# Attention and two mixtures of experts on one core: the second routing, its order on three engines, and the fourth sub-tiles' transfers

## The reference

```python
x = attention(q, k, v)                       # 1536 tokens x 512
# first mixture: top 2 of 8, D=512, F=1024
noisy = x @ w_gate + log1p(exp(x @ w_noise)) * noise
out[mask] += top2_w[mask, k, None] * (relu(x[mask] @ w1[e]) @ w2[e])
# second mixture: top 1 of 8
logits = x @ w_gate + modality_bias[modality_id]
e_idx = argmax(logits); gate_w = softmax(logits)[e_idx]
out[mask] = gate_w[mask, None] * (relu(x[mask] @ w1[e]) @ w2[e])
```

## Time and profile before

| what | us |
|---|---|
| median of 3 runs | 687.44 |
| lowest, highest | 685.09, 689.46 |
| the profiled execution | 682.12 |
| its span, first to last instruction | 680.2 |
| TensorE busy | 645.6 |
| VectorE, ScalarE, GpSimd busy | 322.6, 276.2, 185.5 |
| mean granted TensorE clock | 0.982 |

### The profile page before, as it was taken

One profiled execution on the slowest core, in us unless ns is written; L12 is line 12 of the kernel. 1 busy time (PEld: TensorE's weight loads), 2 busy tenths in 40 slices (PEclk: granted clock), 3 DMA queues, 4 the chain that ended last, 5 costly groups with the idle time before them and its releaser, 6 DMA issues.

```text
span 680.2 us, 11358 instructions
## 1 busy us (share of the span) xinstructions
PE 645.6 (95%) x3872; PEld 585.2 (86%) x3873; DVE 322.6 (47%) x651; ACT 276.2 (41%) x529; POOL 185.5 (27%) x194
## 2 busy tenths in 40 slices
PE   7989999899999999999999999999499999999993
PEld 6989999898999999999999998998278888788873
DVE  4466646587465527254452724353775422452211
ACT  5668866442444234253433523232245221441210
POOL 2500100117361633516153331101531212111101
PEclk9999999999999999999999999998599999999997
DMA  7877822255584545656364511510894510010100
GB/s 207 277 238 244 284 74 68 91 220 134 197 231 162 110 146 154 188 155 172 116 140 151 154 20 22 159 53 8 221 375 156 175 42 31 35 31 32 47 16 27
DMA packets 52096, 91.23 MB, mean 134 GB/s; under 512 B 8591, under 2 KB 14735, under 8 KB 52048
## 3 DMA queue, kind: packets, MB, share of 16 engines
q1 hardware_dynamic: 41872, 69.21, 30.1%
q0 software_dynamic: 10176, 21.38, 13.9%
HBM read 74.52 MB, written 18.40 MB: 137 GB/s over the span
## 4 chain that ended last, share of the span: by engine, by line
PE 83%; DVE 6%; DMA 3%; ACT 2%; issue 2%; SPq 1%; ACTq 0%; POOL 0%; DVEq 0%; POOLq 0%
PE banks L984 6%; PE banks L983 6%; PE banks L992 6%; PE banks L925 5%; PE banks L926 5%; PE banks L928 5%; PE banks L730 5%; PE banks L758 4%; PE banks L1234 4%; PE banks L1239 4%; PE banks L1235 4%; PE banks L1260 4%; PE banks L1261 4%; PE banks L1264 3%; PE banks L742 2%
## 5 line engine op out<-in xcount | busy, mean ns | idle before, releaser
L603 POOL DMA_INDIRECT x_moe<-rows,dst_idx x29 | 57.8, 1994 | 157.5 <-DVE rows L2067 111.2
L1679 DVE TENSOR_TENSOR split<-stage,split 128x2048 fp32r<-128x2048 f32 x32 | 73.3, 2290 | 42.4 <-ACT split L1326 42.3
L925 PE MATMUL banks<-xTs,split 128*128 128x416 f32 (+1 forms) x256 | 88.9, 352 | 2.0 <-issue 2.0
L926 PE MATMUL banks<-xTs,split 128*128 128x416 f32 (+1 forms) x256 | 86.4, 342 | 0.0
L983 PE MATMUL banks<-hTs,split 128*128 128x416 f32 x224 | 80.0, 357 | 0.0
L984 PE MATMUL banks<-hTs,split 128*128 128x416 f32 x224 | 78.6, 351 | 0.0
L1461 ACT ACTIVATE hTs<-banks 128x416 fp32r<-128x416 f32 x56 | 29.0, 518 | 85.0 <-PE banks L928 85.0
L1326 ACT ACTIVATE split<-stage 128x2048 fp32r<-128x2048 f32 x32 | 60.9, 1907 | 0.7 <-DMA stage<-w1a 0.7
L1581 ACT ACTIVATE hTs<-banks 128x512 fp32r<-128x512 f32 x28 | 16.6, 597 | 108.2 <-PE banks L1249 108.2
L928 PE MATMUL banks<-xTs,split 128*128 128x416 f32 (+1 forms) x256 | 56.3, 341 | 0.0
L730 PE MATMUL banks<-k_sb,q_sb 128*128 128x260 f32 (+2 forms) x192 | 50.0, 387 | 3.4 <-DMA k_sb<-k_w 2.0
(11 more groups left out here) (306 smaller groups left out, 1330.0 us busy)
## 6 DMA issues: line engine op xcount, KB each, us to landing
stage<-w1a SPq DMA_DIRECT2D x16, 1024.0 KB, 6.7
stage<-w2a SPq DMA_DIRECT2D x16, 1024.0 KB, 5.6
k_sb<-k_w SPq DMA_DIRECT2D x12, 520.0 KB, 4.7
raw<-w1b SPq DMA_DIRECT2D x6, 1024.0 KB, 6.3
raw<-w2b SPq DMA_DIRECT2D x6, 1024.0 KB, 6.2
q_sb<-q_t SPq DMA_DIRECT2D x24, 128.0 KB, 3.1
x_attention<-rows SPq DMA_DIRECT2D x12, 256.0 KB, 5.6
split<-x_moe SPq DMA_DIRECT2D x12, 256.0 KB, 3.8
```

The costliest lines, as they stand in the source:

```text
L603: pool.indirect_dma_start(out=x_dram[1], out_offset=rows_at(dst_idx[0], early_dst, e, k), in_=y_room(n), in_offset=None, compute_op=ALU.ad ...
L925: pe.matmul(psum, piece(slot, 0, o + c * FH), xTs[:, 0, c, 0:cols], start=(c == 0), stop=False)
L926: pe.matmul(psum, piece(slot, 1, o + c * FH), xTs[:, 0, c, 0:cols], start=False, stop=False)
L1679: dve.tensor_tensor(split_chunk(e % 2, 1, c), staged_chunk(e % 2, c), split_chunk(e % 2, 0, c).bitcast(F32), ALU.subtract).then_inc(low_do ...
```

## The change

It does five things:

1. `turned_scores` makes 12 transposes of 16 columns against the identity; the tile `both` is gone. VectorE adds the two halves with one more operation, ahead of its wait for the one-hot products.
2. `last_to_tokens` moves from behind the fourth `back` to between the second and the third.
3. `pick` writes straight into `chosen` in the second routing. `in_use` and `ntiles` are halves of one tile `pair`, and their running sums are made together. The expert order is computed after the places' base (`place`), not before.
4. The first five gathers of the second mixture take their indices from `src_idx[1]` itself, and SyncE's second pair of loads waits for `slots_ready[1]`.
5. In the first mixture an expert's first 384 tokens take the three full sub-tiles and the rest the fourth, whose gathers, gate gathers and scatters move 32 rows (`lines_of`). `yT` is laid out in one row of columns with the parts in reverse order and 128 zeroed columns behind, so that the fourth transposes and logits may read 128 columns from slot 384 on. `sub_gate` is zeroed once.

```diff
-                    mm = pe.matmul(ps2[:, t, :], lgT[:, t // GROUP, at:at + P], both[:], start=True, stop=True)
+                    mm = pe.transpose(ps2[:, t, :], lgT[:, t // GROUP, at:at + P], ident[0:2 * E, 0:2 * E])
...
             for k in range(SUBS):
+                if k == 2:
+                    last_to_tokens()
                 back(last, k, banks[:, k + 1, :])
-            last_to_tokens()
...
-                link(dve.tensor_tensor(noisy[:], ps2, bias_tok[:], ALU.add))
+                link(dve.tensor_tensor(noisy[:], ps2[:, :, 0:E], bias_tok[:], ALU.add))
+                link(dve.tensor_tensor(noisy[:], ps2[:, :, E:2 * E], noisy[:], ALU.add))
...
-            pick(noisy, 0)
-            link(dve.tensor_copy(chosen[:], onehot[:, 0]))
+            pick(noisy, 0, chosen[:])
...
                     link(dve.tensor_scalar(in_use[:], ntiles[:], 1.0, None, ALU.min))
-                    link(dve.tensor_tensor(cumsq[:], spread(in_use[:], 1, E), upto[:], ALU.mult))
-                    link(dve.tensor_reduce(nth_up_to[:], cumsq[:], AX.X, ALU.add))
-                    link(dve.tensor_tensor(cumsq[:], spread(nth_up_to[:], 1, E), spread(iota_row[:, 0:E], 2, E), ALU.is_le))
+                    link(dve.tensor_tensor(pair_sq[:], spread(pair[:], 2, E), spread(upto[:], 1, 2), ALU.mult))
+                    link(dve.tensor_reduce(pair_up_to[:], pair_sq[:], AX.X, ALU.add))
...
-            sp.wait_ge(src_copied, 2)
+            sp.wait_ge(slots_ready[1], 1)
...
-                pool.tensor_copy(src1[:, b:b + 1], src_idx[1][:, bass.ds(t, 1)]).then_inc(src_copied, 1)
-                gated(pool, "pool", src_copied, t + 1)
+                where = src1[:, b:b + 1]
+                if isinstance(t, int):
+                    where = src_idx[1][:, t:t + 1]
+                else:
+                    pool.tensor_copy(where, src_idx[1][:, bass.ds(t, 1)]).then_inc(src_copied, 1)
+                    gated(pool, "pool", src_copied, t - 4)
...
-                return 1 + SUBS * (e - 1) + (k + 1) % SUBS
+                return 1 + SUBS * (e - 1) + k
+
+            def lines_of(k):
+
+                return slice(0, P if k < SUBS - 1 else SHORT)
...
-                pool.indirect_dma_start(out=x_rows[:, k], out_offset=None, in_=x_dram[0],
+                pool.indirect_dma_start(out=x_rows[lines_of(k), k], out_offset=None, in_=x_dram[0],
```

More of the change, by code:

```diff
@@ L125, in build @@
             row_hot_early = early.enter_context(nc.sbuf_tensor("row_hot_early", [P, EARLY, P], BF16))
-        yT = sb("yT", [P, DC, SLOTS])
-        sinkT = sb("sinkT", [P, P], F32R)
+        with ExitStack() as early:
+            early.enter_context(nc.sbuf_tensor("yT_room", [P, DC * SLOTS], F32))
+            sinkT = early.enter_context(nc.sbuf_tensor("sinkT", [P, P], F32R))
+        yT_wide = sb("yT", [P, DC * SLOTS + P])
+        yT_parts = yT_wide[:, 0:DC * SLOTS].rearrange("p (d n) -> p d n", d=DC)
         with ExitStack() as early:
@@ L179, in build @@
         counts = sb("counts", [P, E, TILES])
-        ntiles = sb("ntiles", [P, E])
-        cum = sb("cum", [P, E])
-        cumsq = sb("cumsq", [P, E, E])
+        pair = sb("pair", [P, 2, E])
+        pair_up_to = sb("pair_up_to", [P, 2, E])
+        pair_sq = sb("pair_sq", [P, 2, E, E])
+        ntiles, in_use = pair[:, 0, :], pair[:, 1, :]
+        cum, nth_up_to = pair_up_to[:, 0, :], pair_up_to[:, 1, :]
+        cumsq = pair_sq[:, 0]
         start = sb("start", [P, E])
-        in_use = sb("in_use", [P, E])
         last_used = sb("last_used", [P, 1])
-        nth_up_to = sb("nth_up_to", [P, E])
         place = sb("place", [P, TILES, E])
@@ L358, in subs_of, with yT_at @@
             return EARLY_SUBS if e == 0 else SUBS
+        def yT_at(d, first, n):
+            o = (DC - 1 - d) * SLOTS + first
+            return yT_wide[:, o:o + n]
         def turned_rows(e, k):
@@ L966, in early_second_low @@
                         pe.wait_ge(h1_low, c + 1)
-                    mm = pe.matmul(psY1[:, d // 2, at:at + EARLY_SLOTS], piece(0, 0, DC * F + c * D + d * P),
+                    mm = pe.matmul(early_y(d), piece(0, 0, DC * F + c * D + d * P),
                                    hTs[:, 1, c, 0:EARLY_SLOTS], start=False, stop=(d % 2 == 1 and c == FC - 1), skip_group_check=True)
@@ L1025, in last_logits @@
                 for k in range(SUBS):
-                    first = min(k * P, SLOTS - P)
-                    mm = pe.matmul(psLast[:, k, :], yT[:, d, first:first + P], wg2[:, d, :], start=(d == 0 and k == 0),
+                    mm = pe.matmul(psLast[:, k, :], yT_at(d, k * P, P), wg2[:, d, :], start=(d == 0 and k == 0),
                                    stop=(d == DC - 1 and k == SUBS - 1), skip_group_check=True)
@@ L1088, in back @@
                     pe.wait_ge(rest_h_low, 2)
-                first = min(k * P, SLOTS - P)
                 for d in range(DC):
-                    mm = pe.transpose(psum[:, d * P:(d + 1) * P], yT[:, d, first:first + P], ident[:])
+                    mm = pe.transpose(psum[:, d * P:(d + 1) * P], yT_at(d, k * P, P), ident[:])
                 mm.then_inc(rows1, 1)
@@ L1852, in over_e, with pick @@
                 return spread(ap, 2, E)
-            def pick(values_, k):
+            def pick(values_, k, hot):
                 link(dve.tensor_reduce(top[:, k, :], values_[:], AX.X, ALU.max))
@@ L1859, in pick @@
                 link(dve.tensor_reduce(keymax[:], ra[:], AX.X, ALU.max))
-                link(dve.tensor_tensor(onehot[:, k], ra[:], over_e(keymax[:]), ALU.is_equal))
+                link(dve.tensor_tensor(hot, ra[:], over_e(keymax[:]), ALU.is_equal))
             def token_rows(unit_rows, away, tokens, n):
@@ L1900, in place_tokens @@
                     link(dve.tensor_scalar(in_use[:], ntiles[:], 1.0, None, ALU.min))
[L1901 to L1903 removed]
+                    link(dve.tensor_tensor(pair_sq[:], spread(pair[:], 2, E), spread(upto[:], 1, 2), ALU.mult))
+                    link(dve.tensor_reduce(pair_up_to[:], pair_sq[:], AX.X, ALU.add))
+                else:
+                    link(dve.tensor_tensor(cumsq[:], spread(ntiles[:], 1, E), upto[:], ALU.mult))
                     link(dve.tensor_reduce(cum[:], cumsq[:], AX.X, ALU.add))
[L1905 to L1909 removed]
                 link(dve.tensor_tensor(start[:], cum[:], ntiles[:], ALU.subtract))
@@ L1921, in place_tokens @@
                                                   psR.rearrange("p (t e) -> p t e", e=E), ALU.mult, ALU.add))
+                    link(dve.tensor_tensor(cumsq[:], spread(nth_up_to[:], 1, E), spread(iota_row[:, 0:E], 2, E), ALU.is_le))
+                    dve.tensor_copy(used[:, m, 1:2], nth_up_to[:, E - 1:E]).then_inc(order_ready, 1)
+                    link(dve.tensor_reduce(order_f[:], cumsq[:], AX.X, ALU.add))
+                    link(dve.tensor_copy(order[:], order_f[:]))
+                    dve.sem_inc(order_ready, 1)
                 places = lg.rearrange("p t (k e) -> p k t e", k=TOP)[:, 0:top_k]
-                link(dve.tensor_tensor(places, spread(place[:], 1, top_k), onehot[:, 0:top_k], ALU.mult))
+                link(dve.tensor_tensor(places, spread(place[:], 1, top_k), (onehot[:], spread(chosen[:], 1, 1))[m], ALU.mult))
                 link(dve.tensor_reduce(pos[:, 0:top_k, :], places, AX.X, ALU.add))
@@ L2074, in second_router @@
                 link(dve.tensor_tensor(wg2_parts[:, :, 1, :], wg2[:], wg2_parts[:, :, 0, :].bitcast(F32), ALU.subtract))
-                dve.wait_ge(ident_ready, 2)
-                link(dve.tensor_tensor(both[:], ident[0:2 * E, 0:E], ident[0:2 * E, E:2 * E], ALU.add))
                 for k in range(2):
```

55 lines of the change are left out of this document (29 added, 26 removed).

## The result

The changed kernel takes **690.44 us** (685.31 to 695.58, 20 runs) beside 686.2 us (684.04 to 689.46, 20 runs) of the kernel before in the same session: ratio 1.0057, 95% interval [1.0034, 1.0079]. Measured twice more, in sessions of their own, it gave 1.0034 [1.0012, 1.0056] and 1.0047 [1.0025, 1.0069]. So it is slower by 0.3 to 0.6%, some 3 us, where 1.6 us faster was predicted, and 690.44 lies above the range.

What follows compares the result with a forecast made beforehand. TensorE was taken as the bound, except for one dependent chain between the MoEs, roughly 470 to 494 us. 3.3 + 0.45 - 2.2 = 1.6 us faster, applied to the median 687.44, gave 685.8 us; range 682.0 to 689.8.

Steps and rivals of the forecast that it cites:

- the term for the fourth sub-tiles of 32 rows: First MoE's gathers, gate gathers and scatters moving a quarter: counted as nothing, since TensorE is dense there.
- What stands ahead of S: Chain until S, the moment the second MoE's list of sources is complete: 3.3 us earlier, between 2.0 and 4.2.
- The turned scores: Turning the scores back before the second routing: 12 transposes replace 12 fp32 products, gain 1.4 us, 0.3 at the other end.
- The one-hot products: Adding the last expert to the scores: waits for 8 transposes, not 16; gain 1.3 us, 1.9 if the clock stays high.
- choice and places: VectorE's expert choice and token placing in the second routing: 0.3 us from a dropped copy, 0.3 from joined running sums.
- rival 3: Change does less before the list of sources (transposes, ranks, GpSimd's wait for scatters): 0.65 us slower, 688.1 us; chance 0.15.
- What stands behind S: From the complete list of sources to the second MoE's first tile: 0.45 us gained, 2.2 us lost.
- the 0.45: First gather of the second MoE: without GpSimd's index copy it starts 0.45 us sooner after the list of sources.
- 2.2 us lost: First gather of the second MoE, behind SyncE's second pair of loads: lands after 6.1 us, not 3.9; ends 0 and 4.9.
- rival 2: First gather stands behind all loads, lands after 8.8 us, clock falls (1.7 us): 2.9 us slower, 690.3 us; chance 0.13.
- decides from a landing of 7.7 us on: Threshold for the first gather's landing, beyond which the case of it standing behind all loads was to decide.
- Rival 1: First gather only shares the DMA engines with the loads: gain 2.9 us, or 3.3; 684.3 us; chance 0.27.

Runs made afterwards that it cites:

- The undone version: Changed kernel with the index copies on GpSimd and SyncE's second pair of loads behind the second copy again, second measurement: ratio 0.9986 to the kernel before.

## Why the prediction was wrong

**The step that failed most is the term for the fourth sub-tiles of 32 rows: "I cost it at nothing".** They cost 3.0 us, at a place that I had not looked at: GpSimd's DRAIN behind the last scatter (in timed runs 3.8 us between the two side by side that differ in these rows alone). Their own effect in the first MoE was nothing, as said: from the first turn back to the stretch it is 278.57 us before and 278.49 after. I took the end of the last product as the end of the program, although the trace of before has 6.7 us behind the last scatter's issue. No row of before could have told that short transfers lengthen the DRAIN; but an unexplained 4.00 us at the very end should have carried a bound.

**What stands ahead of S: right, and undersized.** The turned scores gained 1.93 us, not 1.4: a transposing piece with 16 columns is 0.07 us, below both of my bounds (0.116 and 0.207). The one-hot products gained 1.65, not 1.3; the clock stayed up through the first eight turns back, since the eight turns back took 1.07 us in place of 1.66, so that the split of the logits was nearly the bound, the end that I had given as 1.9. From the end of the one-hot products to S it is 11.88 us, not 12.28: 0.4 of the 0.6 for choice and places. GpSimd's operand, which waited for the scatters, was done at 483.70, 0.43 after `row_hot`; this small loss is the mechanism of rival 3. Starting it early gained nothing when it was tried. S came 1.93 + 1.65 + 0.40 = 3.98 us earlier, and I had written 3.3. (The ends of the four terms add up to 2.1 and 4.1, not the 2.0 and 4.2 that I gave; nothing hangs on it.)

**What stands behind S.** The gather's start at S + 0.33 instead of S + 0.58 gave 0.25 of the 0.45. The landing was put at 6.1 us, and from issue to use it was 6.5, 8.7 and 6.6 in the three profiles: "2.2 us lost" was 2.5 to 4.6. The forecast left out what follows: TensorE without products from 489.4 to 492.1, the clock at 0.50 for 3.4 us on the first tile, which cost 1.70 us. That price was in rival 2, to the tenth, and I had tied it to a landing of more than 7.7 us; it happened at 6.5. **The error is the threshold "decides from a landing of 7.7 us on"**, which I had worked out from when the gather makes the kernel slower, not from when TensorE stands idle. The products without use end 4.1 us after S and the rows are there 6.85 us after it: 2.8 us of idleness, and the clock fell. In the kernel before it was 0.71 us and it did not.

So the balance of the first profile is 3.98 + 0.25 - 2.47 - 1.70 = 0.06 us won in the stretch instead of 1.6. At the end 3.0 are lost. The three profiles average (2.9 + 5.0 + 2.9) / 3 = 3.6 us, the three measurements 3.2 us.

**The rivals.** Rival 1 (the gather shares) fell: q0 moves nothing for 3.3 us. Once packets of the gathers run they do share, 132 to 393 with the loads, as the Trainium skill's rule in "DMA: Bandwidth & Descriptors" (section "Queues, rings and completion order") has it; what comes before the first packet is not in that rule. Rival 2 had the fall of the clock and the right side (690.3 us), though the gather did not stand behind all of the loads: its packets began while theirs still ran; its probability of 0.13 was too low, since the two rows of before with loads ahead had both been slow. It missed the DRAIN and undersold what the chain would win, and these errors cancel: that its time is so close to the measured 690.44 is luck. The undone version shows the price of part 4 alone: 3.5 us between stretches of 30.8 and 34.3. Rival 3's wait for the scatters occurred, and was paid for by larger gains.

## What to carry over

Ahead of a gather on the critical path, hold back bulk loads from another queue until it is issued, or has landed: here the semaphore that SyncE waits for is worth 4 us, as much as the other gains of the change together. A change that hides behind other work in the middle of a program can still show at its end: compare the time from the last transfer to the end of the span too. When a transfer moves, redo the count of what keeps TensorE busy until it lands: here 2.2 to 5.2 us of idleness brought the lower clock on the first tile in 11 profiles of 13.

## What the hardware showed that was not expected

- GpSimd's last DRAIN took 4.00 us in all eight profiles whose indirect transfers had 128 rows, and 6.86 or 6.98 us in all twelve with any shorter. Why transfers that were over nearly 200 us earlier matter is open; only the rows moved were varied.
- A gather issued behind 2 MB of loads moved its first packet 3.5 to 4.8 us later (12 profiles), and its 128 rows were used after 6.3 to 8.7 us. With these loads behind it, it was 1.7 to 2.9 us to the first packet and 3.7 to 5.2 us to the use (8 profiles). What holds the first packet back was not found.
- GpSimd's operand of the codes and VectorE's `row_hot` delayed each other. In the 12 profiles in which GpSimd's began well after `row_hot` but beside it, it took 0.84 to 1.52 us and ended 0.43 us behind `row_hot`, however early it had begun. Where both began together (5 profiles), it took 0.57 us and `row_hot` 2.18 instead of 1.76.
- A semaphore increment that stands behind an indirect DMA in GpSimd's program released SyncE 0.19 us before the engine began that DMA. It is no mark of the DMA's issue; the increment by a copy, or the DMA's own, is.
- Twelve fp32 transposes of 16 x 128 took 0.85 us in 12 pieces (0.07 each), while 12 products of the same rows with 8 columns took 2.78 us in 24.
- The time from the program's start to the stretch differed between profiled executions by up to 10 us (460.6 to 471.0, and 461.8 to 467.6 for the same changed kernel). It includes waits at 160 us without a releaser that the profile shows. It may go in part with the session, since the median of the kernel before moved by 4.7 us between sessions. Its cause was not tried; it is why single profiles don't rank these kernels, and why I compare the stretch and the end.
